# Attention and two mixing layers in one kernel: the prologue put in another order

## The reference

```python
# attention without softmax; 8 heads of 64 columns
kv  = einsum('bhsd,bhse->bhde', k, v)
out = einsum('bhsd,bhde->bhse', q, kv)
x   = out / sqrt(mean(out*out, -1) + 1e-6) * g_norm

# layer 1: low rank mixing over the rows (rank 32), then an MLP
h   = x.T @ U @ V                    # U 576 x 32, V 32 x 576
u   = x + h.T
x2  = u + relu(u @ w_ch1) @ w_ch2    # w_ch1 512 x 2048

# layer 2: gated mixing
h    = gelu(x2 @ w_in); u, v = halves of h
v_n  = (v - mean) / sqrt(var + 1e-6) * g_ln
out2 = x2 + (u * (w_sg @ v_n + b_sg)) @ w_out
```

## Time and profile before

| what | value |
|---|---|
| device time, median of 3 runs | 1294.76 us (1294.64 to 1295.74) |
| device time of the profiled execution | 1293.79 us |
| its span, first to last instruction | 1292.0 us |
| TensorE busy | 1261.8 us, 98% of the span |
| VectorE busy | 824.7 us, 64% |
| ScalarE busy | 543.8 us, 42% |
| GpSimd busy | 101.3 us, 8% |
| mean granted clock of TensorE | 0.993 |

### The profile page before, as it was taken

One profiled execution on the slowest core, in us unless ns is written; L12 is line 12 of the kernel. 1 busy time (PEld: TensorE's weight loads), 2 busy tenths in 40 slices (PEclk: granted clock), 3 DMA queues, 4 the chain that ended last, 5 costly groups with the idle time before them and its releaser, 6 DMA issues.

```text
span 1292.0 us, 21466 instructions
## 1 busy us (share of the span) xinstructions
PE 1261.8 (98%) x8311; PEld 1221.4 (95%) x8311; DVE 824.7 (64%) x1196; ACT 543.8 (42%) x867; POOL 101.3 (8%) x107
## 2 busy tenths in 40 slices
PE   5799999999999999999999999999999999999998
PEld 5699999999999999999999999998898998998987
DVE  4886465645555558998888889976634535336343
ACT  4565454445455445654535444534322212223121
POOL 7210000000000000000000000002302012022000
PEclk9899999999999999999999999999999999999999
DMA  9555665655565456671735446362342241340321
GB/s 236 131 154 154 176 164 157 156 147 156 173 166 157 129 189 242 215 260 62 265 101 191 170 154 225 100 196 57 96 85 66 62 113 50 72 111 31 57 58 41
DMA packets 285365, 178.61 MB, mean 138 GB/s; under 512 B 197456, under 2 KB 255840, under 8 KB 285296
## 3 DMA queue, kind: packets, MB, share of 16 engines
q1 hardware_dynamic: 282336, 172.82, 46.3%
q0 software_dynamic: 1600, 4.56, 1.3%
q10 hardware_dynamic: 1360, 0.30, 0.1%
HBM read 109.47 MB, written 66.06 MB: 136 GB/s over the span
## 4 chain that ended last, share of the span: by engine, by line
PE 93%; DVE 3%; issue 1%; ACT 1%; SPq 1%; DMA 0%; POOL 0%; DVEq 0%; ACTq 0%; POOLq 0%
PE ps L1418 28%; PE ps L1420 28%; PE ps L1419 27%; PE ps L1439 3%; PE ps L1450 2%; PE ps L1423 2%; PE ps L1458 1%; PE ps L1681 1%; PE ps L1684 1%; PE ps L1469 1%; PE ps L1452 1%; DVE w_lo L1180 0%; SPq L376 0%; DVE y L1018 0%; DVE x_lo L1073 0%
## 5 line engine op out<-in xcount | busy, mean ns | idle before, releaser
L1418 PE MATMUL ps<-x_hi,w 128*128 128x288 f32 x896 | 268.0, 299 | 3.5 <-DVE x_lo L1073 2.7
L1419 PE MATMUL ps<-x_lo,w 128*128 128x288 f32 x896 | 264.6, 295 | 0.0
L1420 PE MATMUL ps<-x_hi,w 128*128 128x288 f32 x896 | 264.3, 295 | 0.0
L1418 PE MATMUL ps<-r_hi,w_hi 128*128 128x384 f32 x672 | 224.6, 334 | 0.1
L1420 PE MATMUL ps<-r_hi,w_lo 128*128 128x384 f32 x672 | 224.5, 334 | 0.0
L1419 PE MATMUL ps<-r_lo,w_hi 128*128 128x384 f32 x672 | 224.5, 334 | 0.0
L880 ACT ACTIVATE r_hi<-hb 128x768 fp32r<-128x768 f32 x168 | 142.4, 848 | 168.5 <-PE ps L1420 164.7
L1418 PEld LDWEIGHTS ps<-x_hi,w 128*128 128x128 f32 x896 | 168.5, 188 | 5.6 <-issue 4.3
L1420 PEld LDWEIGHTS ps<-x_hi,w 128*128 128x128 f32 x896 | 168.8, 188 | 0.0
L1419 PEld LDWEIGHTS ps<-x_lo,w 128*128 128x128 f32 x896 | 168.7, 188 | 0.0
L1208 DVE TENSOR_TENSOR r_lo<-hb,r_hi 128x768 fp32r<-128x768 f32 x120 | 114.5, 955 | 30.0 <-ACT r_hi L880 30.0
(11 more groups left out here) (156 smaller groups left out, 2347.1 us busy)
## 6 DMA issues: line engine op xcount, KB each, us to landing
hT_scratch<-h_st SPq DMA_DIRECT2D x64, 576.0 KB, 4.6
hb<-hT_scratch SPq DMA_DIRECT2D x24, 1536.0 KB, 7.5
uT_scratch<-x_raw SPq DMA_DIRECT2D x32, 288.0 KB, 2.3
x_st<-uT_scratch SPq DMA_DIRECT2D x24, 384.0 KB, 3.5
x2T_scratch<-x_st SPq DMA_DIRECT2D x24, 384.0 KB, 7.0
x_raw<-x2T_scratch SPq DMA_DIRECT2D x8, 1152.0 KB, 5.6
xt_in<-x2T_scratch SPq DMA_DIRECT2D x144, 64.0 KB, 2.5
k_raw<-in_k SPq DMA_DIRECT2D x64, 128.0 KB, 4.0
```

The source lines that it names most:

```text
L1418: mm(dst, ws[0], xs[0], start=first, stop=False, skip_group_check=chained)
L1419: mm(dst, ws[0], xs[1], start=False, stop=False, skip_group_check=chained)
L1420: return mm(dst, ws[1], xs[0], start=False, stop=last, skip_group_check=chained)
```

## The change

Only the prologue and the first steps of up tile 0 change.

- **Loads.** SyncE loads k and v of units 0 to 4 and q of unit 4. ScalarE issues q of units 0 and 1, GpSimd q of units 2 and 3, between V and w_ch1. GpSimd loads U before it clears kv and V_aug. The tail of k of unit 0 waits for five memsets instead of 13.
- **Stores.** uT(0) and uT(1) are stored ahead of unit 5's k and v, uT(2) ahead of its q blocks.
- **Table.** ScalarE runs one sqrt before the first copy.
- **TensorE.** Twelve transposes of the identity into an unused bank run ahead of unit 0. q is transposed ahead of k·v.
- **Low rank of units 0 to 3** is in fp32: U_rep holds U three times and zeros in the fourth place, y isn't split. `low_rank_factors` forms U_aug from U_rep after the first normalisation.
- **Order of ScalarE.** In units 0 to 3, `q_copy` of the next unit stands ahead of `std`.
- **VectorE.** `w1_low(1)` moves into the loop over the units; the pieces of unit 4 (`sums`, `normalise`, `y_low`) stand between the first sums and remainders of x, and `w1_sums` of group 1 behind them.
- **Unit 4.** Its attention runs in the prologue, and k·v of unit 5 behind step 1 instead of step 0.
- **w_ch1** is loaded in its second and third part behind k·v of units 3 and 4 instead of 2 and 3. GpSimd's sums also wait for those of VectorE (`s_wsum[1]`).

```diff
     # SyncE
-                if m == 0:
-                    sp.wait_ge(s_zero, 1 + 3 * HP)
+                if m < 2:
+                    sp.wait_ge(s_zero, 5 if m == 0 else 2 + 3 * HP)
...
             for m in range(1, HP):
                 load_kv(0, m, m, m)
-                load_q(0, m, m, m)
             load_kv(1, 0, HP, 0)
             load_q(1, 0, HP, 0)
             store_u(0, 0)
-            load_next(HP + 1)
-            for r in range(1, HP):
-                store_u(0, r)
+            store_u(0, 1)
+            load_kv((HP + 1) // HP, (HP + 1) % HP, HP + 1, 0)
+            store_u(0, 2)
+            load_q_blocks(HP + 1)
+            store_u(0, 3)
     # GpSimd
+            pool.dma_start(U_raw[:, 0:JM, :], ...).then_inc(s_ul, 16)
+            pool.dma_start(U_raw[0:ST, JM, :], U[SM:S, :]).then_inc(s_ul, 16)
             nc.gpsimd.memset(kv[:], 0.0).then_inc(s_zero, 1)
             nc.gpsimd.memset(V_aug[:, S:].bitcast(F32), 0.0).then_inc(s_zero, 1)
+            nc.gpsimd.memset(U_rep[:, :, 3 * R:], 0.0).then_inc(s_zero, 1)
             for n in range(4):
                 pool.dma_start(V_raw[R * n:R * (n + 1), :], V[:, :]).then_inc(s_small, 16)
+            for m in range(2, HP):
+                for h in range(2):
+                    pool.dma_start(q_raw[m][:, 0:JM, h, :], ...).then_inc(s_q[m], 16)
+                pool.dma_start(q_raw[m][0:ST, JM, :, :], ...).then_inc(s_q[m], 16)
...
             pool.wait_ge(s_kv, 1)
             load_w1(0, slice(0, 2))
-            pool.wait_ge(s_kv, 3)
+            pool.wait_ge(s_kv, HP)
             load_w1(1, slice(2, 4))
-            pool.wait_ge(s_kv, HP)
+            pool.wait_ge(s_kv, HP + 1)
             load_w1(2, slice(4, NPAIR))
+            pool.wait_ge(s_wsum[1], 4)
     # ScalarE
+                if m == 0:
+                    act.wait_ge(s_zero, 1)
+                    nc.scalar.activation(stdv[:, 0:1], eps_col[:], ACT.Sqrt).then_inc(s_pass, 1)
...
                 attn_copy(m, BX, BY, ym)
                 squares(m, sq_first, ym)
+                q_copy(m + 1, 0)
+                q_copy_tail(m + 1, 1)
+                std(m)
                 if m > 1:
                     u_evacuated(m - 2, m - 2, 4, 0, -1)
-                std(m)
-                q_copy(m + 1, 0)
-                q_copy_tail(m + 1, 1)
-                if m:
-                    a_part(m - 1, 3)
-                y_high(m, ym)
-                if m > 1:
                     w1_high(m - 2)
             x_high(0, 0, 0)
             u_evacuated(2, 2, 4, 0, -1)
-            a_part(3, 3)
             x_high(0, 0, 1)
+            attn_copy(HP, BX, BY)
             u_evacuated(3, 3, 4, 0, -1)
+            squares(HP, sq)
+            def first_steps():
+                x_high(0, 0, 2)
+                copied(0, 1)
+                std(HP)
+                x_high(0, 0, 3)
+                kv_copy(HP + 1, BY, P)
+                copied(0, 3)
+                x_high(0, 0, 4)
+                y_high(HP)
+                x_high(0, 0, 5)
+                copied(0, 5)
+                x_high(0, 0, 6)
     # VectorE
+            U_repeated()
             kv_copy(0, 2)
-            low_rank_factors()
             for m in range(HP):
                 ym = y_first[m % 3]
                 sums(m, sq_first)
                 kv_copy(m + 1, 2)
+                if m == HP - 1:
+                    a_split_first(m - 1)
                 normalise(m, ym)
-                if m:
-                    a_split(m - 1, 3)
-                y_low(m, ym)
+                if m == 0:
+                    low_rank_factors()
+                elif m < HP - 1:
+                    a_split_first(m - 1)
                 if m == 1:
                     w1_sums(dve, nc.vector, 0)
-                if m == 2:
-                    w1_low(0)
+                elif m > 1:
+                    w1_low(m - 2)
             x_sum(0, 0, 1)
-            a_split(3, 3)
-            w1_low(1)
+            a_split_first(3)
             x_low(0, 0, 0)
-            for idx, low_ in ((2, 1), (6, 2), (4, 3)):
-                x_sum(0, 0, idx)
-                x_low(0, 0, low_)
+            x_sum(0, 0, 2)
+            x_low(0, 0, 1)
+            sums(HP, sq)
+            x_sum(0, 0, 6)
+            x_low(0, 0, 2)
+            normalise(HP)
+            x_sum(0, 0, 4)
+            x_low(0, 0, 3)
+            y_low(HP)
+            x_low(0, 0, 4)
             w1_sums(dve, nc.vector, 1)
     # TensorE
+            def low_rank_first(m):
+                pe.wait_ge(s_y, m + 1)
+                for j in range(NJ):
+                    ins = mm(ps[:, 3, 0:P], U_rep[:, j], y_first[m % 3][:, j], start=(j == 0), stop=(j == NJ - 1))
+                ins.then_inc(s_a, 1)
...
+            for n in range(WARM):
+                ins = transpose(ps[:, 4, 0:P], identF[:], True, True)
             q_k_v_first(0)
             for m in range(HP):
...
                 q_k_v_first(m + 1)
                 if m:
-                    low_rank(m - 1, 3)
+                    low_rank_first(m - 1)
             pe.wait_ge(s_uev, 2)
             u_transposed(2, 4, y_first[2])
-            low_rank(3, 3)
+            low_rank_first(3)
+            pe.wait_ge(s_o, 2 * HP)
+            attention(HP, BX, BY)
             pe.wait_ge(s_uev, 3)
             u_transposed(3, 4, y_first[0])
...
-                if first and k == 0:
-                    attention_and_next(m)
+                if first and k == 1:
+                    pe.wait_ge(s_o, 2 * (HP + 1))
+                    k_v(HP + 1, BY, 1, 2, P)
```

More of the change, by code:

```diff
@@ L54 @@
 NO = NJ
+WARM = 12
 NXT = 3
@@ L152, in build @@
     q_raw = [q_raw] + [at(f"q_raw{i}", [P, NJ, 2, HD], F32) for i in range(1, HP)]
-    y_first = [y] + [at(f"y{i}", [P, NJ, P], F32) for i in range(1, 3)]
+    y_first = [at(f"y{i}", [P, NJ, P], F32) for i in range(1, 3)] + [y]
     sq_first = at("sq_first", [P, NJ, P], F32)
-    U_raw = at("U_raw", [P, NJ, R], F32)
-    V_raw = at("V_raw", [P, S], F32)
+    U_rep = at("U_rep", [P, NJ, 4 * R], F32)
     assert cursor[0] <= phase_end
+    V_raw = at("V_raw", [P, S], F32, offset=x_hi_off + 2 * SH * 4)
+    U_raw = at("U_raw", [P, NJ, R], F32, offset=x_hi_off + 3 * 2 * SH * 4)
     wsize = FH * DH * 4
@@ L817, in _ @@
             u_evacuated(2, 2, 4, 0, -1)
-            a_part(3, 3)
             x_high(0, 0, 1)
+            attn_copy(HP, BX, BY)
             u_evacuated(3, 3, 4, 0, -1)
-            for idx in range(2, NI):
-                x_high(0, 0, idx)
+            squares(HP, sq)
             X_HIGH_AT = (26, 34, 53)
             X_HIGH_THEN = (1, 2, 3, 6)
+            def first_steps():
[10 more added lines that the diff above has]
+                x_high(0, 0, 6)
             def up_tile(t, par, first=False, end=False):
-                for k in range(STEPS):
+                if first:
+                    first_steps()
+                for k in range(6 if first else 0, STEPS):
                     g, idx, s_ = step(k)
@@ L1031, in a_split, with a_split_first, U_repeated @@
                 nc.vector.tensor_tensor(a_aug[o, :], part[o, :], a_aug[o, :].bitcast(F32), ALU.subtract).then_inc(s_alo, 1)
+            def a_split_first(m):
+                a = ps[:, 3, 0:P]
+                dve.wait_ge(s_a, m + 1)
+                nc.vector.tensor_copy(a_aug[:], a).then_inc(s_ahi, 1)
+                dve.wait_ge(s_ahi, m + 1)
+                o = slice(R, 2 * R)
+                nc.vector.tensor_tensor(a_aug[o, :], a[o, :], a_aug[o, :].bitcast(F32), ALU.subtract).then_inc(s_alo, 1)
+            def U_repeated():
+                dve.wait_ge(s_ul, 32)
+                for n in range(3):
+                    nc.vector.tensor_copy(U_rep[:, :, R * n:R * (n + 1)], U_raw[:]).then_inc(s_urep, 1)
             def low_rank_factors():
-                dve.wait_ge(s_small, 16 * 6)
-                for n in range(3):
-                    nc.vector.tensor_copy(U_aug[:, :, R * n:R * (n + 1)], U_raw[:]).then_inc(s_lowt, 1)
+                dve.wait_ge(s_urep, 3)
+                nc.vector.tensor_copy(U_aug[:], U_rep[:]).then_inc(s_lowt, 1)
+                dve.wait_ge(s_small, 16 * 4)
                 nc.vector.tensor_copy(V_aug[:, 0:S], V_raw[:]).then_inc(s_lowt, 1)
-                dve.wait_ge(s_lowt, 4)
+                dve.wait_ge(s_lowt, 2)
                 nc.vector.tensor_tensor(U_aug[:, :, 3 * R:4 * R], U_raw[:], U_aug[:, :, 0:R].bitcast(F32), ALU.subtract).then_inc(s_low, 1)
@@ L1123, in up_tile @@
             def up_tile(t, par, first=False, end=False):
-                for k in range(STEPS):
+                for k in range(5 if first else 0, STEPS):
                     g, idx, s_ = step(k)
@@ L1139, in up_tile @@
                         a_split(m, BX)
-                    if k in X_LOW_THEN[2 if first else 0:]:
+                    if k in X_LOW_THEN[3 if first else 0:]:
                         x_low(t, par, 2 + X_LOW_THEN.index(k))
@@ L1485, in _ @@
                 if m > 1:
+                    if m == 2:
```

(3 more changed lines are left out.)

43 lines of the change are left out of this document (23 added, 20 removed).

## The result

The changed kernel took 1297.94 us (median of 20 runs, 1295.47 to 1300.3); the kernel before took 1294.77 (20 runs) beside it. The ratio is 1.0023, with a 95% interval of 1.0016 to 1.0030: slower by 3 us, where 7 us faster was forecast. The profiled execution has a span of 1294.8 us.

The account below looks back on a forecast made before the run. TensorE is busy from unit 5's attention (67.14 us) on, so only its start counts: 6.2 us gained at step 0, 2.1 within the tile, 1.1 given back to the clock, 7.1 in sum; 1287.7 us, range 1282 to 1292.

Parts of the forecast that it names:

- signs of being wrong: w_ch1 sums find data at once and early start carries through; step 0 awaits another transfer; stretch behind unit 5's attention changes.
- Start: Unit 0: earlier tails, early sqrt table and 12 transposes bring its attention from 12.96 to roughly 9.5 us; costed at nothing.
- GpSimd's queue: Prologue: six q loads, 4.8 us for two units, delay w_ch1's first part, issued by 17.8 and landing at 23.1 us.
- VectorE's order: Prologue: group 0's w_ch1 sums stand ahead of unit 2's; unit 3's attention starts at 27.3 us instead of 29.65.
- To the first up step: From unit 3's attention to step 0, which starts at 39.75 us instead of 45.93: 6.2 us gained.
- First up tile: k·v of unit 5 at 42.0 us with 0.65 stall; VectorE's ten operations until 48.0; unit 5's attention at 58.9.
- Clock: Before unit 5's attention: one TensorE stretch at 1.2 GHz costs 1.1 us, moving that attention to 60.0.
- Rival 2: DMA engines bind and three queues bring nothing; w_ch1's first part lands at 25.2; gain 4 us, 1290.8; chance 0.17.
- Rival 1: First up tile: VectorE's chain doesn't bind, unit 5's attention starts at 54.2; 1281.8 us, halfway 1284; chance 0.18.
- Rival 4: Prologue: q loads delay w_ch1's first part, making unit 3's attention later; 1297.5 us if landing is at 33; chance 0.04.

Follow-up runs that it names:

- e2: Changed kernel with only the third part of w_ch1 moved later, issued behind k·v of unit 5 instead of unit 4: 1286.05 us, 0.9933 of the kernel before.
- e1: Changed kernel with second and third part of w_ch1 issued behind k·v of units 2 and 3 again: 1291.52 us, 0.9978 of the kernel before.
- e9: Changed kernel with 32 unused identity products on TensorE ahead of the wait for unit 5's k and v: 1295.36 us, 1.0002 of the kernel before.
- e7: e2 without the 12 transposes that run ahead of unit 0: 1286.34 us, 0.9928 of the kernel before.
- e10: e2 without the early sqrt on ScalarE: 1287.17 us, 0.9935 of the kernel before.
- e8: Changed kernel with w_ch1's second part behind unit 2's k·v and third behind unit 5's: 1286.38 us, 0.9938 of the kernel before.
- e12: e2 with q of units 1 to 3 issued by SyncE again: 1288.55 us, 0.9950 of the kernel before.

## Why the prediction was wrong

**The step that failed.** It is the one for k·v of unit 5 in the first up tile: "with 5 to 6 us of landing it starts at 42.0 and ends at 43.1, a new stall of 0.65". The v took 12.1 us, TensorE stood still for 7.72 us, and k·v ran from 49.09. The landing time is that of the kernel before, where unit 5's k and v took 4.5 to 5.7 us, and the third part of w_ch1 was issued 8 us ahead of them (26.90 and 34.85). The diff moves its gate from unit 3's k·v to unit 4's, which in the changed kernel falls at 32.7 us, 1.4 us ahead of them. In the working part by part this edit doesn't appear at all. It stood in the list of edits, and it had no price. None of the prediction's signs of being wrong named a wait at k·v of unit 5 either. e2, which moves only that gate, comes out at 0.9933; the forecast was a gain of 7.1 us of 1294.8, or 0.9945, inside e2's interval. That isn't a full acquittal of the rest, since e2 puts the third part later than either kernel. With the parts exactly where they were (e1), the time is 0.9978: unit 5's v lands as assumed there, but the store of uT(1) doesn't, 7.7 us against the 5.7 allowed, and the clock falls. The forecast thus took landing times from a traffic that neither the changed kernel nor e1 has. The order of work it assumed is that of e2. That its sum is only 1.6 us too cautious there is partly luck: unit 5's attention starts 2.7 us earlier than the 60.0 forecast, and the stretch behind it, which was to stay at 1224.9 us, takes 1226.3.

**Where the 12.3 us between the profiles of the changed kernel and e2 lie** (unit 5's attention at 69.62 and at 57.33; 1.1 of them are given back behind it). The first 8.0 are the start of its k·v, 49.09 and 41.11. From there to the attention the changed kernel needs 20.5 us and e2 16.2. e9 splits these 4.3: with TensorE kept busy it needs 18.1, so 2.4 are the clock that fell in the wait. The other 1.9 weren't taken apart by a run. The traces show two things there: the wait for the split of unit 4 is 2.79 us in e9 and 1.29 in e2, and the steps behind it run at half clock in e9 and not in e2. The split's last row takes 1.25 us in e9 and in the changed kernel, where GpSimd's sums run beside it, and 0.28 in e2, where they come later; no run moves these sums alone. The prediction held the clock for 1.1 us in all.

**Step by step.**
- *Start* costed at nothing: right. e7 and e10 show no difference without transposes or early sqrt, e7 with unit 0's k·v at 2.34 us. Both were tried in e2 only, and the memset waits weren't undone.
- *GpSimd's queue*: right. Forecast landing 23.1, measured 24.0; the q loads were cheaper (0.78 for a pair's half instead of 0.92), so the issue ended at 17.3.
- *VectorE's order*: right to 0.7 us at its end, with an error inside that had room. Unit 2's attention starts at 21.49 and not at 18.8, as its v was late, and VectorE stands at the w_ch1 sums for 1.20 us and not for 2.8.
- *To the first up step*: 39.60 against 39.75.
- *First up tile*: wrong in its first sentence. The rest of it is tested by e2, where nothing is late: attention 5 at 57.33 against 58.9. VectorE's chain reached the w_ch1 sums at 48.41 (forecast 48.0). The stretched x_lo of 1.84 us didn't come, because GpSimd's sums had to wait for their data (the profiles of e8, e10 and e12, with the same late gate, name the loads of w_ch1). In the changed kernel, where they began at 60.48, they met the split of unit 4 and not the x_lo.
- *Clock*: right that it costs, too small for a wait of 8 us.

**The rivals.** Rival 2 had the right resource, the wrong mechanism and a price of 3 us instead of 11.6. I looked for a delay of w_ch1's first part, and had the last 2.1 MB cost "some 1 us". What I held against it, "the needed bytes are put ahead of those that aren't needed yet", isn't so for this part: the diff puts it right ahead of unit 5's loads. Its rule, from the Trainium skill (DMA: Bandwidth & Descriptors, "Issuing engines are not separate DMA queues"), says that transfers of all queues interleave, and this trace agrees: 72% and 29% for two queues at once, from which the loss starts. Its other half, that several queues only save issue time, isn't decided here: e12 is 2.2 us slower by the ratios, with overlapping intervals and with w_ch1's first part moved as well. Rival 1 (VectorE's chain doesn't bind) is half borne out by e2: unit 5's attention at 57.33 lies between its 54.2 and the forecast's 58.9, and TensorE still waits 1.8 us for two x_lo and 1.3 for the split of unit 4. Rival 4, the one for slower, had the wrong transfer: w_ch1's first part, where it was the third. That its 1297.5 meets the measured 1297.9 is chance.

**What stays open.** Why the changed kernel's own runs spread over 5 us and those of the kernel before over 3 wasn't tested; the profiles show stretches at half clock at different places. Nor was it tested why GpSimd's queue gets more of the DMA engines than SyncE's; its packets were larger (1.02 MB in 310, against 0.37 MB in 745). The low rank in fp32 wasn't undone alone.

## What to carry to other kernels

A load's landing time depends on what else is in flight (2.7, 5.5 and 12.1 us here for the same v in e2, e1 and the changed kernel), so when a change moves the gate of a large transfer, ask which small, urgent transfers will now be issued right behind it; they pay for it. Price every edit of a diff, the moved constants in waits too: of some twenty edits here, one number decided the sign (1.0023 against 0.9933). And a gain at the start of a chain counts only where the chain arrives: 6.3 us at step 0 were gone two steps later.

## What the runs showed of the hardware that was not expected

- With GpSimd's queue loaded, issuing on SyncE was slowed as well as landing: the four q block issues took 9.87 us on SyncE in the changed kernel and 2.28 in e2.
- A wait of 8 us on TensorE cost more than itself. e9 ran 64 matmul rows of no use (7.3 us) and came out 2.7 us faster than the changed kernel.
- Transposes can raise TensorE's clock, by the durations (the granted clock in the profile reads 1.00 there with and without them). With the twelve fp32 transposes ahead, 2.82 us in all, unit 0's k·v took 1.28 to 1.35 us in seven of ten profiles and 1.73 to 1.92 in the other three; without them (e7) it took 2.34, as before (2.47). It was of no use here, since the loads came later anyway.
